# A fused attention and mixture-of-experts kernel: every load of an expert's weights in four pieces

## The reference

```python
# 1: attention both ways between 512 rows and 32 state rows, per batch and head
a  = softmax(x @ state.T / 8);  xread = a @ state
a2 = softmax(state @ x.T / 8);  sread = a2 @ x
x  = concat([xread, sread]).reshape(4352, 512)
# 2: a dense layer
h = x @ w_in                                  # (512, 2048)
x = (h * clip(h + 3, 0, 6) / 6) @ w_out       # (2048, 512)
# 3: eight experts, each row goes to the one with the largest logit
e = argmax(x @ w_gate, axis=1)
out[row] = gate_w * eom * (relu(x[row] @ w1[e]) @ w2[e])   # w1[e] (512, 1024), w2[e] (1024, 512)
```

## Time and profile before

| | |
|---|---|
| median of 3 runs | 1168.76 us (1167.61 to 1173.7) |
| the profiled execution, own time | 1167.76 us |
| its span, first to last instruction | 1166.0 us |
| mean granted TensorE clock | 0.988 |
| TensorE busy | 1127.7 us |
| VectorE, ACT, POOL busy | 639.4, 466.8, 76.8 us |
| moved by DMA | 131.36 MB |
| loads of an expert's weights | 14 of 2048 KB, 11 by ACT and 3 by SP |

### The profile page before, as it was taken

How to read it: one execution, slowest core, us unless ns; L and a number is a source line. 1 busy time by engine, 2 the same in 40 slices (tenths; PEclk the granted TensorE clock), 3 DMA queues, 4 the chain that set the end, 5 groups by cost and what they waited for, 6 DMA issues and landing times.

```text
span 1166.0 us, 20895 instructions
## 1 busy us (share of the span) xinstructions
PE 1127.7 (97%) x6358; PEld 886.0 (76%) x6359; DVE 639.4 (55%) x1247; ACT 466.8 (40%) x780; POOL 76.8 (7%) x96
## 2 busy tenths in 40 slices
PE   9999999999999999999999988989999999979995
PEld 7777777777777777777778977777888888858884
DVE  6675654655646556556564347557464435556632
ACT  4554434443444444434544351435342223344420
POOL 0000100101001001010010110010011010100000
PEclk9999999999999999999999989999999999989998
DMA  9210110101001100110020275677675444856442
GB/s 375 80 37 10 64 37 37 40 34 74 37 1 73 37 37 37 37 73 1 1 109 1 79 258 182 205 274 228 191 261 169 146 144 128 284 161 208 156 140 63
DMA packets 98783, 131.36 MB, mean 113 GB/s; under 512 B 13967, under 2 KB 75023, under 8 KB 94352
## 3 DMA queue, kind: packets, MB, share of 16 engines
q1 hardware_dynamic: 91360, 89.35, 23.7%
q10 hardware_dynamic: 1584, 23.07, 5.5%
q0 software_dynamic: 5760, 17.90, 4.0%
HBM read 85.86 MB, written 45.47 MB: 113 GB/s over the span
## 4 chain that ended last, share of the span: by engine, by line
PE 85%; DVE 4%; issue 3%; DMA 2%; SPq 2%; ACTq 2%; ACT 1%; DVEq 0%; POOL 0%; POOLq 0%
PE y_ps L855 33%; PE h_ps L837 15%; PE y_ps L928 13%; PE y_ps L912 7%; PE h_ps L912 6%; PE a_ps L812 2%; PE h_ps L827 2%; DMA hid_mv<-hidden 1%; ACTq L444 1%; DVE we L483 1%; PE a_ps L715 1%; PE a_ps L796 1%; PE a_ps L776 1%; DMA hidden<-expert_hid 1%; SPq L574 1%
## 5 line engine op out<-in xcount | busy, mean ns | idle before, releaser
L855 PE MATMUL y_ps<-w_out_hi,hid_hi 128*128 128x512 f32 x544 | 218.6, 402 | 0.0
L855 PE MATMUL y_ps<-w_out_lo,hid_hi 128*128 128x512 f32 x544 | 213.0, 392 | 0.0
L855 PE MATMUL y_ps<-w_out_hi,hid_lo 128*128 128x512 f32 x544 | 212.6, 391 | 0.0
L928 PE MATMUL y_ps<-we,act_t_hi 128*128 (+1 forms) x608 | 187.9, 390 | 4.4 <-issue 2.6
L1365 DVE SCALAR_TENSOR_TENSOR hid<-hid,h_ps 128x512 f32<-128x512 f32 (+1 forms) x144 | 94.4, 656 | 168.2 <-ACT hid L1035 168.2
L837 PE MATMUL h_ps<-att_hi,mix 128*128 128x512 f32 x512 | 184.5, 403 | 0.1
L1035 ACT ACTIVATE hid<-h_ps,three 128x512 f32<-128x512 f32 (+1 forms) x144 | 95.4, 662 | 177.4 <-PE h_ps L837 154.0
L855 PEld LDWEIGHTS y_ps<-w_out_hi,hid_hi 128*128 128x128 f32 x544 | 102.1, 188 | 51.1 <-issue 30.4
L928 PEld LDWEIGHTS y_ps<-we,act_t_hi 128*128 128x128 f32 x608 | 113.9, 188 | 30.3 <-issue 6.1
L1374 DVE TENSOR_TENSOR hid_lo<-hid,hid_hi 128x512 fp32r<-128x512 f32 (+1 forms) x144 | 94.8, 658 | 70.5 <-ACT hid_hi L1043 70.0
L1552 DVE STREAM_TRANSPOSE act_raw<-hid_mv 128x512 f32<-128x512 f32 x76 | 49.5, 690 | 132.7 <-DMA hid_mv<-hidden 131.3
(11 more groups left out here) (216 smaller groups left out, 1410.9 us busy)
## 6 DMA issues: line engine op xcount, KB each, us to landing
raw<-in_w ACTq DMA_DIRECT2D x11, 2048.0 KB, 8.4
hidden<-expert_hid SPq DMA_DIRECT2D x76, 256.0 KB
hid_mv<-hidden SPq DMA_DIRECT2D x152, 128.0 KB, 2.9
xg<-buckets SPq DMA_DIRECT2D x164, 64.0 KB, 1.9
xb<-in_x_rows SPq DMA_DIRECT2D x8, 1024.0 KB, 4.9
x_t<-in_x_t SPq DMA_DIRECT2D x7, 1024.0 KB, 5.0
buckets<-pad_row SPq DMA_DIRECT2D x8, 774.0 KB, 8.5
raw<-in_w SPq DMA_DIRECT2D x3, 2048.0 KB, 8.1
```

Source lines behind the costliest of these rows:

```text
L855: i = pe.matmul(y_ps[:, t, :], (hid_hi, hid_lo)[hp][:, hid_at(b, j), t * P:(t + 1) * P], w_out_s[wp][:, j, :], start=(j == 0 and m == 0), ...
L928: i = pe.matmul(y2_ps[:, slot % 2, :], act_t[hp][:, slot % 2, f, :], we[:, bass.ds(w_at + (wp * WPART + KD * F + f * DM), DM)], start=(f = ...
```

## The change

Each load of an expert's weights was one DMA of 2 MB. It becomes four DMAs of 512 KB, each with 4 KB of every partition, issued one behind the other by the same engine at the same place. Each adds 16 to the semaphore, so that every wait is for 64 per load in place of 16, that is, for all four pieces.

```diff
+    def load_pieces(eng, w, raw, weights):
+
+        for i in range(PIECES):
+            eng.dma_start(raw[:, i * PIECE:(i + 1) * PIECE], weights[:, i * PIECE:(i + 1) * PIECE]
+                          ).then_inc(sem(f"raw{w + 1}_loaded"), 16)
...
-        sp.dma_start(raw1[:], w1[0].rearrange("p k f -> p (k f)")).then_inc(sem("raw1_loaded"), 16)
+        load_pieces(sp, 0, raw1, w1[0].rearrange("p k f -> p (k f)"))
...
-        sp.dma_start(raw2[:], w2[0].rearrange("p j d -> p (j d)")).then_inc(sem("raw2_loaded"), 16)
+        load_pieces(sp, 1, raw2, w2[0].rearrange("p j d -> p (j d)"))
...
-        sp.dma_start(raw1[:], w1[bass.ds(e, 1)].rearrange("o p k f -> p (o k f)")).then_inc(sem("raw1_loaded"), 16)
+        load_pieces(sp, 0, raw1, w1[bass.ds(e, 1)].rearrange("o p k f -> p (o k f)"))
...
-        sp.wait_ge(sem("raw1_loaded"), 16 * 2)
-        sp.wait_ge(sem("raw2_loaded"), 16 * 2)
+        sp.wait_ge(sem("raw1_loaded"), 16 * PIECES * 2)
+        sp.wait_ge(sem("raw2_loaded"), 16 * PIECES * 2)
...
-            wait(act, f"raw{w + 1}_loaded", 16 * (n + 1))
+            wait(act, f"raw{w + 1}_loaded", 16 * PIECES * (n + 1))
...
-            act.dma_start(raw1[:], w1[bass.ds(e, 1)].rearrange("o p k f -> p (o k f)")
-                          ).then_inc(sem("raw1_loaded"), 16)
+            load_pieces(act, 0, raw1, w1[bass.ds(e, 1)].rearrange("o p k f -> p (o k f)"))
...
-            act.dma_start(raw2[:], w2[bass.ds(e, 1)].rearrange("o p j d -> p (o j d)")
-                          ).then_inc(sem("raw2_loaded"), 16)
+            load_pieces(act, 1, raw2, w2[bass.ds(e, 1)].rearrange("o p j d -> p (o j d)"))
```

## The result

The changed kernel takes 1185.01 us (median of 4 runs, 1183.63 to 1187.03), the kernel before beside it 1169.45 us: a ratio of 1.0129, 95% interval 1.0098 to 1.0161, or 15.6 us slower. I had forecast 1177 and a loss of 8.4 us. The sign was right and the time lies in the stated range, but the forecast loss was about half of the measured one. The ratios in this document come from the runs of a kernel and of the kernel before beside it; a difference of two medians can differ from its ratio by 1 to 2 us. Of all executions one, of a later variant (w2's load behind `hidden_hi`), took 2263.3 us for a reason that I don't know; its ratio leaves it aside.

What follows compares the result with a forecast made beforehand. TensorE, busy 97% of the span, was taken as the bound, so only its idle holes count. Issues 10.9, relief -3.4 and clock 1.9 sum to +9.4 us on 1167.76, giving 1177; range 1165 to 1187.

Steps and rivals of the forecast that it cites:

- The issues on ACT: ACT's queue at changes of expert: three more pieces cost 1.5 us a load, +10.9 us in all.
- B: Change of expert with loads at 755.76 and 762.38, TensorE hole ahead of 764.74: issues cost 3.1 us, no cover.
- C: Next change of expert, TensorE hole of 2.05 us ahead of 811.34: issues cost 3.1 us, no cover.
- D: Change of expert where TensorE takes its tile at 866.68: 1.5 us of cover leaves 1.6 us of issue cost.
- the clock: TensorE behind the grown hole at C: lower granted clock slows a tile, +1.9 us.
- relief: Hidden writes at B and E: 4 KB packets let them through the load sooner, 1.7 us each, -3.4 us.
- hole E: TensorE's 7.64 us hole ahead of 1029.13: late expert_hid and hidden add 3.1 us, packets give back 1.7 us.
- hid_mv at 733: SP's transfer at 732.91, 7.59 us beside a load: no gain taken, expected to stay above 6 us.
- No relief: Rival: engines move a load ahead of everything whatever its packets; +12.8 us, 1180.6; chance 0.1.
- ACT's issues blocking: Rival: w2's issues on ACT block at B, C, D and the later E; +18.6 us, 1186.4; chance 0.08.
- Faster: Rival: hid_mv and hidden back at 2.9 us, issues hidden under waits; about 1161; chance 0.07.
- not slower: Rival: shorter waits of hid_mv and hidden, up to 9.5 us, pay for the issues; 1165.2 or 1169.2; chance 0.2.

Runs made afterwards that it cites:

- the paired runs: ACT's loop of two tiles in place of four, with the four pieces (ratio 1.0080) and with whole loads (ratio 1.0012), each against the kernel before.
- The kernel with the added code alone: Kernel before plus seven more issues per tile body under a condition that never holds: 1179.63 us, ratio 1.0071.
- the control with whole loads: Kernel before, whole loads, with ACT's loop turned over two tiles in place of four: 1172.46 us, ratio 1.0012.
- the short loop: Changed kernel, all loads in four pieces, with ACT's loop turned 16 times over two tiles: 1181.47 us, ratio 1.0080 to the kernel before.
- strided pieces: Short loop with four issues per load, each every fourth partition with its whole 16 KB: 1187.14 us, ratio 1.0142 to the kernel before.

## Why the prediction was right in sign and short in size

- **The issues on ACT,** as far as they are executed, were sized well. Four took 1.83 to 2.48 us at B and C against 0.34, so 1.5 us a load, 1.7 for w1 at B, and 2.1 for w1 at C, whose fourth piece took 0.96 us. B came 2.81 us late (3.1 forecast), and the paired runs give 8 us for the pieces in all, where my sum for them was 9.4. That these are so near is in part luck: the sum holds 1.6 us at D that did not come and too little for the clock. Put beside the table above, by place: B 3.1 forecast and 2.8 found, from there to C 1.4 (3.1 less 1.7 of relief) and 7.2, behind C 1.9 and 2.8, D 1.6 and 0, hole E 1.4 and 1.4, behind E 0 and 3.2; together 9.4 and 17.4.
- **The step that failed is "The issues on ACT": it prices what the added instructions take to execute and leaves out the length they add to ACT's loop.** At C it should have had 4.9 us more: ACT needs 5.10 us at the jump, 0.2 before. With it the two issue terms there make 2.1 + 1.5 + 4.9 = 8.5 us, and 7.2 were measured from B to C; the other 1.3 us are mostly hidden's wait, below. The kernel with the added code alone, and the one with the code shortened, show the cause from both sides. The trace of before held a hint: no instruction packet in 260 us of looping, which says that the loop fitted, and a fit can be lost. The Trainium skill, "Runtime: NRT & Kernel Launch", section "Instruction fetch mechanics", states that a taken branch to instructions outside a window of two 16 KiB pages has to fetch them before it goes on. The stall of 5.10 us at the back edge agrees with it; where exactly the limit lies no run here shows.
- **The relief was wrong in its mechanism, and the sum hid it.** The sign that I had named came true, hidden at E under 6 us (5.59), but not by the packets: 4 KB in one issue left it at 8.64 us, and 16 KB in four issues had 5.32. What I booked as relief is an absorption: hidden lands 10.55 us behind w2's first issue before and 10.21 after, so that the 1.5 us which w2's pieces put between the two are waited off anyway. At E w2's first issue stood 16.95 us ahead of the hole before (1004.54 to 1021.49) and 15.43 us after (1018.87 to 1034.30): w1's 1.5 us is what is left, and the hole is 1.42 us longer. I had 3.1 - 1.7 = 1.4 us, the right number for the wrong reason.
- **hid_mv at 733** I took to stay, and it did: the transfer takes 8.08 us (7.59 before), and the hole behind it is 1.86 us (1.46 before).
- **D: 1.6 us forecast, none found.** Behind C TensorE was late itself: the 4.59 us that ACT was idle ahead of its split at D ended with TensorE, and w1's pieces, issued in that time, cost nothing. The cover was larger than the trace of before showed, because the delay ahead of it had made it so.
- **The clock: 1.9 us forecast, some 5 us found on the chain.** TensorE's row is busy 6.9 us longer. Some 2 us of that lie between B and C, under SP's chain, as I had said. From C to the start of hole E TensorE has no hole and takes 2.8 us longer; the granted clock over 820 to 840 is 0.81, where it was 1.00. Behind E it is 1.0 us more, and the last tile's matmuls lose 1.5 us (7.25 in place of 5.73 us) behind a hole of 3.27 us. I had counted C alone. Not all of this need belong to the change: I had read from one execution that the clock stays whole behind holes of 3.04 and 2.05 us, and the control with whole loads had 0.85 behind a hole of 2.96 us, and TensorE busy for 1133.4 us, 5.7 us more than before. How much of the 5 us the change causes is open. Hole C is 6.9 us long by the stall: without its 4.9 us it would be about 2, as in the kernel before, and the short loop shows 2.70.
- **Rivals.** No relief (1180.6) was true as to the relief. ACT's issues blocking did not happen beyond one piece of 0.96 us. Faster, or not slower, had nothing for it.

That hole C of the short loop with pieces is only 2.70 us fits the same account. From B to C it takes 48.90 us against 46.60 before, 2.3 us more, but TensorE works for 46.20 of them against 44.55, at the lower clock behind B, so that only 0.65 us are added to the hole.

What stays open: what makes strided pieces slower besides their issues; how long exactly the loop may be; and how much of the clock's loss is the change's.

## What to carry to other kernels

Ahead of adding instructions to an unrolled device loop, look whether the instruction queues are silent inside it; if they are, as here over 260 us, a few more instructions can bring fetches in each turn whether they are executed or not. Shorten the loop (fewer tiles per turn) before making its body longer. A transfer's issue belongs on an in-order queue where nothing urgent stands behind it: moving the whole load behind expert_hid won 0.4%, cutting it in four in front of it lost 1.3%, of which some 0.5% was the fetch.

## What the hardware showed that I had not expected

- Never executed instructions cost 0.7%: 344 listed instructions in ACT's loop against 304, 69 instruction packets against 32, one stall of 5.71 us on the chain. The longest stall is in each such kernel at the jump right behind an issue of w2's load (5.10, 5.71 and 6.61 us, and 8.28 with the slow blocks of 32 partitions); at the others it was 3.4 us at most. That the fetch waits behind the load is a guess that no run tested.
- A load of 32 neighbouring partitions is slow: 2 MB in four such blocks held the DMA engines 8.5% of the span against 5.6% for four blocks of every fourth partition, at the same 2112 packets.
- A 256 KB write issued 3.1 to 4.6 us behind the first issue of a 2 MB load of another queue landed 10.2 to 12.1 us behind that issue, 1.2 and 1.6 us behind the load where its landing can be read, with packets of 16 KB and with packets of 4 KB.
- At the same place, behind holes of 3.04 and 2.96 us, the granted clock over the next 20 us was 1.00 in one execution of whole loads and 0.85 in another.
